# The 1e-9 of the softmax denominators as an extra row of the last V product, in a sparse attention and mixture-of-experts kernel

## What is computed

```python
scores = scale * np.matmul(q, k.transpose(0, 1, 3, 2))
kth = np.partition(scores, -top_k, axis=-1)[..., -top_k:-top_k + 1]
scores = np.where(scores >= kth, scores, -1000000000.0)
attn = np.exp(scores - np.max(scores, axis=-1, keepdims=True))
attn = attn / (np.sum(attn, axis=-1, keepdims=True) + 1e-09)
attn_out = np.matmul(attn, v)
...
# for each of the two chosen experts e of a token, with weight top2_w:
h = np.maximum(x[mask] @ w1[e], 0.0)
out[mask] += top2_w[mask, k, None] * (h @ w2[e])
```

## Time and profile before

| | us |
|---|---|
| median of 3 runs | 1311.79 |
| lowest and highest | 1311.41 and 1312.60 |
| the profiled execution | 1312.3 |
| its span (first to last instruction) | 1310.6 |
| VectorE busy in the span | 920.3 (70%) |
| TensorE busy | 1089.4 (83%) |
| GpSimd busy | 741.2 (57%) |
| ScalarE busy | 585.2 (45%) |
| mean granted TensorE clock | 0.919 |

### The profile page before, as it was taken

How to read it: one execution, slowest core, us unless ns; L and a number is a source line. 1 busy time by engine, 2 the same in 40 slices (tenths; PEclk the granted TensorE clock), 3 DMA queues, 4 the chain that set the end, 5 groups by cost and what they waited for, 6 DMA issues and landing times.

```text
span 1310.6 us, 20173 instructions
## 1 busy us (share of the span) xinstructions
PE 1089.4 (83%) x5919; PEld 902.8 (69%) x5920; DVE 920.3 (70%) x1790; ACT 585.2 (45%) x1249; POOL 741.2 (57%) x602
## 2 busy tenths in 40 slices
PE   4777777787876787777778389999999999999997
PEld 3556666676665666666667278878888888788886
DVE  7999999999999999999998862425242424242221
ACT  3555556555555555555555342424242424242221
POOL 4878777778787778787874113334343433342222
PEclk7988898889889988887998589999999999999999
DMA  7502210221122012201200144343333424211120
GB/s 236 167 10 55 55 31 25 55 55 29 27 55 55 23 33 55 55 15 41 55 10 14 37 172 166 110 136 109 131 124 123 140 96 163 78 56 62 54 66 1
DMA packets 78047, 97.63 MB, mean 74 GB/s; under 512 B 47839, under 2 KB 47839, under 8 KB 77986
## 3 DMA queue, kind: packets, MB, share of 16 engines
q1 hardware_dynamic: 67346, 66.12, 16.6%
q0 software_dynamic: 10320, 30.16, 7.1%
q10 hardware_dynamic: 320, 0.59, 0.2%
HBM read 79.80 MB, written 20.71 MB: 77 GB/s over the span
## 4 chain that ended last, share of the span: by engine, by line
DVE 54%; PE 31%; DMA 10%; issue 2%; POOL 2%; ACT 1%; POOLq 0%; DVEq 0%; SPq 0%
DVE work L722 23%; DVE top L728 21%; PE ps_o L1126 14%; PE ps_h L1100 12%; DVE top L714 7%; DMA out<-y_sb,out_rows 4%; DMA prev<-out,out_rows 3%; DMA xin<-x_dram,tile_rows 2%; PE ps_s L1111 2%; PE ps_x L1083 1%; PE ps_o L1034 1%; POOL out_rows L490 1%; DVE y_sb L919 1%; DVE o_rec L750 0%; DVE W L850 0%
## 5 line engine op out<-in xcount | busy, mean ns | idle before, releaser
L1034 PE MATMUL ps_o<-vA,pT 128*128 128x128 f32 (+3 forms) x1600 | 282.6, 322 | 58.0 <-ACT pT L596 57.9
L452 POOL TENSOR_SCALAR probs<-scores,top 128x576 f32<-128x576 f32 x142 | 244.7, 1723 | 140.8 <-DVE top L728 113.9
L1034 PEld LDWEIGHTS ps_o<-vA,pT 128*128 128x128 f32 (+3 forms) x1600 | 227.1, 204 | 116.0 <-ACT pT L596 88.4
L728 DVE MAX8 top<-work 128x8 f32<-128x576 f32 x432 | 304.6, 746 | 0.0
L1126 PE MATMUL ps_o<-W,hh 128*128 x688 | 223.9, 397 | 5.2 <-DVE hl L904 5.2
L1100 PE MATMUL ps_h<-W,xh 128*128 (+1 forms) x688 | 224.7, 398 | 1.4 <-DVE xl L883 1.4
L722 DVE MATCH_REPLACE8 work<-top,work 128x576 f32<-128x576 f32 x288 | 211.6, 742 | 0.0
L456 POOL TENSOR_TENSOR probs<-probs,expd 128x576 f32<-128x576 f32 x142 | 199.8, 1407 | 11.8
L1009 PE MATMUL ps_p<-ident,probs 128*128 128x128 f32 x576 | 106.0, 313 | 110.1 <-POOL probs L456 108.7
L919 DVE SCALAR_TENSOR_TENSOR y_sb<-ps_o,slot_weight,prev 128x512 f32<-128x512 f32 x43 | 32.3, 751 | 220.5 <-PE ps_o L1126 116.3
L501 POOL DMA_INDIRECT out<-y_sb,out_rows x43 | 52.2, 1213 | 214.3 <-DVE y_sb L919 205.6
(11 more groups left out here) (146 smaller groups left out, 1630.1 us busy)
## 6 DMA issues: line engine op xcount, KB each, us to landing
raw<-w SPq DMA_DIRECT2D x16, 2048.0 KB, 9.3
q_raw<-q_t SPq DMA_DIRECT2D x64, 144.0 KB, 2.9
k_raw<-k_t SPq DMA_DIRECT2D x60, 144.0 KB, 3.0
out<-zeros SPq DMA_DIRECT2D x18, 256.0 KB
vA<-v SPq DMA_DIRECT2D x32, 128.0 KB, 2.4
x_dram<-o_fin SPq DMA_DIRECT2D x32, 128.0 KB, 2.2
xin<-x_dram,tile_rows POOLq DMA_INDIRECT x43, 3.4
prev<-out,out_rows POOLq DMA_INDIRECT x43, 3.3
```

The costliest lines, as they stand in the source:

```text
L452: nc.gpsimd.tensor_scalar(probs[:, s % PRING, :], scores[:, s % RING, :], top[:, s % RING, ROUNDS - 1, 7:8], None, ALU.is_ge).then_inc(mas ...
L728: nc.vector.max(top[:, r, n + 1, :], work[:, a, :])\
L1034: mm = nc.tensor.matmul(ps_o[a:z, 0:P], pT[0:rows, s % 2, c * P + a:c * P + z], vA[u][0:rows, h, c, :], start=(c == 0), stop=(c == KB))
```

## The change

Row 64 of the last block (one row beyond the 64 keys of the rest) is put to use. In `pT` it holds 1.0, in `vA` it holds zeros in V's columns and 1e-9 (`EPS`) in column 64, the column of the sums; the zeros behind that column were there before. The last product of each output tile takes 65 rows, so that its column 64 is the sum plus 1e-9. The reciprocals are formed from `o_raw` directly, `o_rec` has one value a tile in place of two, and the semaphores `norm_step` and `last_step` count once a call in place of twice. The new rows are filled once, by VectorE, ahead of its first work; `ones_ready` then counts to 10 in place of 4, and SyncE's V loads and TensorE's first matmul wait for that.

```diff
--- before.py
+++ after.py
@@ -22,6 +22,7 @@
 TOP_K = 32
 ROUNDS = TOP_K // 8
 STEPS = 2 * ROUNDS - 3
+EPS = 1e-9
 
 
 def sparse_attention_moe_kernel(
@@ -134,7 +135,7 @@
         o_raw = sb("o_raw", [P, 2, QT, HD + 1])
         top = sb("top", [P, RING, ROUNDS, 8])
         neg_max = sb("neg_max", [P, RING, 1])
-        o_rec = sb("o_rec", [P, 2, QT, 2])
+        o_rec = sb("o_rec", [P, 2, QT])
         zeros = sb("zeros", [P, D])
 
         split = sb("split", [P, 4 * (S + HD) + 8 * S], F32R)
@@ -337,7 +338,7 @@
 
             for h in range(2):
                 load_raw(sp, q_raw[h], q_t, 0, h)
-            sp.wait_ge(ones_ready, 4)
+            sp.wait_ge(ones_ready, 10)
             for u in range(2):
                 load_v(u, u)
             for h in range(2):
@@ -431,13 +432,13 @@
 
             def normalise(i, u, first=False):
 
-                pool.wait_ge(norm_step, 2 * (2 * i + u) + 2)
+                pool.wait_ge(norm_step, 2 * i + u + 1)
                 if not first:
 
                     pool.wait_ge(x_out[u], 64 * i + 1)
                     pool.wait_ge(o_turned, 3 * (2 * i + u - 1))
                 nc.gpsimd.tensor_tensor(o_fin[:, u, :, :], o_raw[:, u, :, 0:HD],
-                                        o_rec[:, u, :, 1:2].to_broadcast([P, QT, HD]), ALU.mult).then_inc(norm_done, 1)
+                                        o_rec[:, u, :].unsqueeze(2).to_broadcast([P, QT, HD]), ALU.mult).then_inc(norm_done, 1)
 
             def body(i, first, last):
                 for s in range(BODY):
@@ -747,20 +748,22 @@
                 pair = 2 * i + u
 
                 dve.wait_ge(o_copied, QT * (pair + 1))
-                nc.vector.tensor_scalar(o_rec[:, u, :, 0], o_raw[:, u, :, HD], 1e-9, None, ALU.add).then_inc(norm_step, 1)
-                dve.wait_ge(norm_step, 2 * pair + 1)
-                nc.vector.reciprocal(o_rec[:, u, :, 1], o_rec[:, u, :, 0]).then_inc(norm_step, 1)
+                nc.vector.reciprocal(o_rec[:, u, :], o_raw[:, u, :, HD]).then_inc(norm_step, 1)
 
             def last_rows(n, j0, j1):
 
                 dve.wait_ge(o_copied, QT * (PAIRS - 1) + j1)
-                nc.vector.tensor_scalar(o_rec[:, 1, j0:j1, 0], o_raw[:, 1, j0:j1, HD], 1e-9, None, ALU.add).then_inc(last_step, 1)
-                dve.wait_ge(last_step, 2 * n + 1)
-                nc.vector.reciprocal(o_rec[:, 1, j0:j1, 1], o_rec[:, 1, j0:j1, 0]).then_inc(last_step, 1)
-                dve.wait_ge(last_step, 2 * n + 2)
+                nc.vector.reciprocal(o_rec[:, 1, j0:j1], o_raw[:, 1, j0:j1, HD]).then_inc(last_step, 1)
+                dve.wait_ge(last_step, n + 1)
                 nc.vector.tensor_tensor(o_fin[:, 1, j0:j1, :], o_raw[:, 1, j0:j1, 0:HD],
-                                        o_rec[:, 1, j0:j1, 1:2].to_broadcast([P, j1 - j0, HD]), ALU.mult).then_inc(last_norm, 1)
-
+                                        o_rec[:, 1, j0:j1].unsqueeze(2).to_broadcast([P, j1 - j0, HD]), ALU.mult).then_inc(last_norm, 1)
+
+            for u in range(2):
+                nc.vector.memset(pT[KREST:KREST + 1, u, KB * P:(KB + 1) * P], 1.0).then_inc(ones_ready, 1)
+                nc.vector.memset(vA[u][KREST:KREST + 1, :, KB, 0:HD], 0.0).then_inc(ones_ready, 1)
+            dve.wait_ge(ones_ready, 8)
+            for u in range(2):
+                nc.vector.memset(vA[u][KREST:KREST + 1, :, KB, HD:HD + 1], EPS).then_inc(ones_ready, 1)
             dve.wait_ge(qk_hi, 1)
             rest = qS[0][0][0:HD, 0:S]
             nc.vector.tensor_tensor(rest, q_raw[0][0:HD, :], rest, ALU.subtract).then_inc(first_lo, 1)
@@ -989,6 +992,7 @@
 
             pe.wait_ge(consts_ready, 10)
             pe.wait_ge(pads_ready, 4)
+            pe.wait_ge(ones_ready, 10)
             pe.wait_ge(first_lo, 2)
             for g in range(AHEAD):
                 make_scores(0, g, g, True, ps_p if g % 2 else ps_s)
@@ -1030,7 +1034,7 @@
                     parts = [(0, P, j // (MID + 1))] if j != MID else [(0, HD, 0), (HD, P, 1)]
                     for a, z, h in parts:
                         for c in range(KB + 1):
-                            rows = P if c < KB else KREST
+                            rows = P if c < KB else KREST + 1
                             mm = nc.tensor.matmul(ps_o[a:z, 0:P], pT[0:rows, s % 2, c * P + a:c * P + z],
                                                   vA[u][0:rows, h, c, :], start=(c == 0), stop=(c == KB))
                     mm.then_inc(o_done, 1)
```

## The result

| | before | after |
|---|---|---|
| median, us | 1313.47 (8 runs) | 1305.47 (8 runs) |
| lowest to highest, us | 1311.41 to 1319.72 | 1304.33 to 1308.96 |
| ratio of the two | | 0.9943, 95% interval 0.9932 to 0.9955 |
| profiled execution: span, us | 1310.6 | 1303.3 |

The changed kernel is 0.57% faster (0.45 to 0.68%), some 7.5 us. The prediction said 1305.1 us. Its sum was 6.7 us; the two profiled spans differ by 7.3 us. The medians differ by 8.0 us, since the five later executions of before were longer than the three that the prediction started from (1311.79 us).

What follows compares the result with a forecast made beforehand. VectorE was taken to bound the first stage and TensorE the last. The terms, -6.5 - 0.18 + 0 + 0 + 0 = -6.7 us, taken from 1311.8 us, gave 1305.1 us, with a range of 1303.2 to 1308.9 us.

Steps and rivals of the forecast that it cites:

- Part 1: VectorE's search: removing fifteen additions (line 750) saves 0.42 us each, 0.67 us for the slow one, 6.5 us in all.
- Theory (a): Line 750's addition is slow because it competes with GpSimd for SBUF access; the reciprocal need not pay, so 0.42 us goes.
- (b): Whatever stands first behind a MAX8 pays; the reciprocal inherits 218 ns, saving only 3.4 us, 1308.4 us in all; 12%.
- The shut-out of the reciprocal: In the search the reciprocal waits for GpSimd's mask to end, +0.92 us in each of fourteen calls, about 1324 us; 3%.
- Part 2: Tail: four additions (line 757) go; only the last call is on the chain, saving 0.18 us.
- Part 3: Last V product of each output tile: a 65th row costs 0, with 0.4 us to either side.
- Part 4: Start: six fills and three longer waits cost 0, as VectorE is idle until 6.84 us.
- Part 5: TensorE's cold stretches behind 692.9 us may shift: taken as 0, with 1.5 us to either side.
- The rival built on it: Cold stretches over the tail's V products and behind 725 us give back 3 to 6 us, about 1310.5 us; 5%.
- The turn of the chain: End of the search: the chain passes from VectorE to GpSimd at about 686.4 us in place of 692.94.

Runs made afterwards that it cites:

- e7: Kernel before with a second addition, into a tile nobody reads, behind each of the fifteen: 1313.34 us, ratio 0.9998.
- e3: Changed kernel with the addition put back fifteen times, behind the reciprocal, into a tile nobody reads: 1308.63 us, ratio 0.9961 to the kernel before.
- e4: Kernel before with the addition moved between the last two MAX8 of the search pair: 1308.95 us, ratio 0.9960.
- e6: Kernel before with the 64-row product of each output tile put first instead of last: 1314.54 us in a single execution.
- e2: Changed kernel without the 65th row and its fills, additions still gone: 1306.02 us, ratio 0.9939 to the kernel before.
- e5: Changed kernel with rows 64 to 127 filled and the last product at 128 rows: 1305.25 us, ratio 0.9938 to the kernel before.
- e9: Changed kernel with 32 unread matmuls before the first expert tile and 43 in attention's last seven steps: 1310.96 us, ratio 0.9967 to the kernel before.

## Why the prediction was right

**What bounds the kernel.** VectorE bounds the search, and all that is taken from it there reaches the end: search -6.75 us, span -7.3 us.

**Part 1, the fifteen additions.** Foreseen 6.5 us, found 6.75. The price by starts (0.42 us a call) was the right one but for 0.02 us, and the duration (382 ns) was close to it by chance; e7 shows that the two are not the same thing. The 0.02 us a call is the MAX8 that now follows 0.11 us, not 0.13 us, behind the reciprocal. Theory (a), taken because of one instruction that ended with a GpSimd instruction, is shown by e3, e4 and e6; (b), with 12%, is ruled out. The shut-out of the reciprocal did not occur in any of the fifteen calls.

**Part 2, the tail's addition.** 0.18 us foreseen; 11.67 against 11.85 us in e2 and e4. In after the last reciprocal is followed by the product 0.20 us later (714.76 to 714.96 us), where addition and reciprocal took 0.38 (721.30 to 721.68 us in the chain of before).

**Part 3, the row.** Mis-sized, and the reason was wrong. I took 0 with 0.4 us to either side; it is worth 0.5 us in a warm tail. The sign is that of the earlier trace rows, which had the dearer 64-row form in plain view; I treated the gap of 30 ns as a bound and not as the value, because 64 is nearer to 65 than to 128. e5 shows that the distance in rows is not what counts, and the starts of e6 that the cost is that of changing the form, which a 65-row product does not do.

**Part 4, the start.** As foreseen: the fills are over at 2.2 us.

**Part 5, the clock.** Too small. I allowed 1.5 us; a cold tail costs 5 to 7. The rival built on it had 3 to 6 us and 5%. In the profiled pair the clock took 1.6 us in the tail of after (12.8 against 11.2). The tail of before took 0.7 us more than e4's (12.5 against 11.85), although its clock was 1.00 all through: TensorE entered it with a group of V products still to do, behind the cold stretch at 702 us. And after gained 0.4 us at the first expert products (7.08 against 7.47 us): +0.5 us net. That is the size of part 3 with the other sign, so two terms that were both set at 0 nearly cancel in the total. This is luck, and so is part of the last digit: the prediction subtracted 6.7 us from a median of three executions, 1311.8 us, where eight gave 1313.5, and by the ratio the change brings some 7.5 us.

**The turn of the chain.** Wrong in detail. I expected the chain to leave VectorE at about 686.4 us. It stayed there until the last search pair:

```profile
704.54 0.10 DVE top L729
...
705.77 0.82 DVE probs L739
```

In before the chain left earlier; the twenty V matmuls of the middle tile took 4.42 us, in after 2.02 us. That is the clock's work and not the row's: in e2 and e4, with 64 rows but at 2.4 GHz, they took 2.82 us and the chain stayed on VectorE until the last search pair too, while in e3, with the row and a cold stretch from 703.5 us on, it left VectorE at the end of the pair before the last. With TensorE at 2.4 GHz, and without the extra matmuls of e9, VectorE's search is the bound to its end.

## What to carry to other kernels

Price a small instruction on a full engine by the starts of its neighbours, not by its duration, and ask what GpSimd runs beside it: here the same addition cost 0.42, 0.23 or 0.07 us of VectorE's time depending on its place. If it can't be removed, move it ahead of the instruction that lets GpSimd start. And where a stage's end hangs on TensorE's clock, compare stretches between fixed marks and not only total times, since one cold tail hides a change of this size.

## What the runs showed that I had not expected

- Among V products of 128 rows one of 65 or 128 rows is quicker than one of 64, since TensorE does not change form: ten matmuls take 1.38 us in place of 1.57 at 2.4 GHz, 2.50 in place of 2.80 at 1.2 GHz, and the twenty of a split tile 2.02 in place of 2.82. TensorE's busy time fell by 41 us.
- GpSimd's mask (`tensor_scalar` on a 128x576 tensor, 1.72 us) holds back a VectorE addition only until 0.76 us from its start; its subtraction (two SBUF tensors, 1.42 us) until its end.
- A second addition behind the first cost nothing, as the wait for the first one's result was there already.
- The tail of attention takes 11.4 to 11.9 us with TensorE at 2.4 GHz and up to 18.0 us in cold stretches. 32 matmuls that nobody reads, before the first expert tile, were enough to have it warm in the one profile, and brought nothing.
